# Four experts in fixed order and four ranked, with the early gates alone in the DMA queues and attention rows written into the output rows

## The reference

```
for t in range(768):                       # gated linear attention, per batch and head
    m_new = max(f[t] + m, i[t]);  fs = exp(f[t] + m - m_new);  is = exp(i[t] - m_new)
    C = fs * C + is * outer(v[t], k[t]);  n = fs * n + is * k[t]
    y[t] = sigmoid(o[t]) * (C @ q[t]) / max(|n @ q[t]|, 1)
x = y as rows                              # (3072, 320)
logits = x @ w_gate                        # 8 experts; each row goes to its argmax
out[rows of e] = softmax weight * (relu(x[rows of e] @ w1[e]) @ w2[e])     # 320 -> 1024 -> 320
h = out @ w_in;  result = max(0.01 * h, h) @ w_out                         # 320 -> 2048 -> 320
```

## Time and profile before

| | us |
|---|---|
| median of 3 runs (lowest, highest) | 835.92 (832.53, 836.61) |
| the profiled execution | 834.39 |
| its span | 832.7 |
| busy: PE / DVE / ACT / POOL | 746.0 / 531.0 / 388.3 / 146.5 |
| TensorE clock granted, mean | 0.976 of full |

### The profile page before, as it was taken

One profiled execution on the slowest core, in us unless ns is written; L12 is line 12 of the kernel. 1 busy time (PEld: TensorE's weight loads), 2 busy tenths in 40 slices (PEclk: granted clock), 3 DMA queues, 4 the chain that ended last, 5 costly groups with the idle time before them and its releaser, 6 DMA issues.

```text
span 832.7 us, 17702 instructions
## 1 busy us (share of the span) xinstructions
PE 746.0 (90%) x6435; PEld 552.7 (66%) x6436; DVE 531.0 (64%) x1382; ACT 388.3 (47%) x713; POOL 146.5 (18%) x202
## 2 busy tenths in 40 slices
PE   0798999898178899999999989999999999999994
PEld 0577888787157788887888855555555555555552
DVE  7468999898776656766476666555455465554441
ACT  2457464664625557545654323343343433433432
POOL 4334443344131111111010000020010100100101
PEclk9999999999589999999999999999999999999998
DMA  9559999992052995397540000000000000000000
GB/s 235 150 151 307 296 298 288 275 282 83 9 150 95 327 348 198 125 357 271 190 152 2 2 2 2 1 32 1 1 33 1 24 8 0 31 0 1 32 2 31
DMA packets 49401, 99.75 MB, mean 120 GB/s; under 512 B 7822, under 2 KB 38222, under 8 KB 46766
## 3 DMA queue, kind: packets, MB, share of 16 engines
q1 hardware_dynamic: 39906, 67.65, 26.9%
q10 hardware_dynamic: 6780, 22.10, 7.8%
q0 software_dynamic: 2640, 9.01, 3.2%
HBM read 74.85 MB, written 23.89 MB: 119 GB/s over the span
## 4 chain that ended last, share of the span: by engine, by line
PE 81%; DMA 6%; DVE 5%; issue 3%; SPq 2%; ACT 1%; POOL 1%; ACTq 0%; DVEq 0%
PE bank L1524 33%; PE bank L1658 19%; PE bank L1558 12%; PE bank L1391 4%; PE bank L1420 3%; DMA vv<-v_in 2%; DMA d_parts<-xreg 1%; PE bank L1412 1%; PE bank L1514 1%; PE bank L1404 1%; PE bank L1443 1%; PE bank L1381 1%; PE bank L1383 1%; DMA d_x<-og 1%; PE bank L1635 1%
## 5 line engine op out<-in xcount | busy, mean ns | idle before, releaser
L1524 PE MATMUL bank<-stage,slot 128*128 128x512 f16 x768 | 181.1, 379 | 0.0
L1658 PE MATMUL bank<-slot,dec 128*128 128x320 f16 x768 | 159.1, 299 | 0.0
L1524 PE MATMUL bank<-qbd,slot 128*128 128x128 f16 x1984 | 120.1, 223 | 11.1 <-issue 11.1
L1524 PEld LDWEIGHTS bank<-qbd,slot 128*128 128x128 f16 x1984 | 116.2, 100 | 14.2 <-issue 13.9
L1524 PEld LDWEIGHTS bank<-stage,slot 128*128 128x128 f16 x768 | 75.1, 98 | 74.3 <-DVE stage L1323 0.2
L1327 DVE TENSOR_TENSOR qk<-stage,dec 128x512 f16<-128x512 f32 x96 | 66.4, 692 | 84.8 <-ACT dec L853 84.8
L1658 PE MATMUL bank<-slot,qk 128*128 128x320 f16 x384 | 114.8, 299 | 0.0
L1323 DVE TENSOR_TENSOR stage<-bank,stage 128x512 f32<-128x512 f32 x96 | 66.2, 690 | 67.4 <-ACT stage L847 66.9
L853 ACT CAST dec<-stage 128x512 f16<-128x512 f32 x96 | 59.4, 619 | 100.7 <-PE bank L1658 72.8
L1658 PEld LDWEIGHTS bank<-slot,dec 128*128 128x128 f16 x768 | 75.1, 98 | 44.3 <-DVE qk L1327 0.2
L1558 PE MATMUL bank<-slot,emov 128*128 128x320 f16 x496 | 102.0, 299 | 2.3 <-issue 1.5
(11 more groups left out here) (260 smaller groups left out, 1126.4 us busy)
## 6 DMA issues: line engine op xcount, KB each, us to landing
slot<-d_w SPq DMA_DIRECT2D x12, 1280.0 KB, 7.0
d_w<-slot ACTq DMA_DIRECT2D x4, 2560.0 KB, 8.9
stage<-wB SPq DMA_DIRECT2D x6, 1280.0 KB, 7.2
stage<-wA SPq DMA_DIRECT2D x6, 1024.0 KB
d_w<-slot SPq DMA_DIRECT2D x4, 1280.0 KB, 8.9
stage<-wB ACTq DMA_DIRECT2D x4, 1280.0 KB, 14.3
qk<-qkT SPq DMA_DIRECT2D x12, 360.0 KB
slot<-qkT SPq DMA_DIRECT2D x12, 360.0 KB
```

The lines of the kernel that those rows point to most:

```text
L1524: ins = t_.matmul(pf, a[:, col:col + P], x(k), start=(q == 0), stop=(q == len(ops) - 1))
L1658: ins = t_.matmul(bank[4 + q][:, 0:DM], x[f % 2][:, q * P:(q + 1) * P], slotB[2 + f // NF][:, c0:c0 + DM], start=(f == 0 and z == 0), stop ...
```

## The change

- **Start.** SP issues the keys, queries and values of steps 0 and 1, then their output gates, and then waits until step 1's inputs, the exponent parts among them, have landed. Only then come the inputs of steps 2 and 3, with unit 2's first half between them, then `w_gate` and unit 2's second half. DVE's chain fills 128 columns of ones instead of 768 before it starts, and clears `esta` after the parts rather than before. POOL's clearing of the third buffer (`late_set(2)`) waits for that.
- **Rows.** From step 4 on (`EARLY = 4`) POOL writes the finished row into its own columns of `xreg`; PE reads it and SP stores it from there. The output gates of step 8 and later need only that the row is made. ACT clears `xreg` once all rows are stored.
- **Four fixed, four ranked.** `NS = 4`: experts 0 to 3 are fixed, 4 to 7 ranked. Attention converts units 2, 1 and 0 and stores unit 2 alone; unit 3 is squared in attention and converted after it; unit 4 (the first ranked one) is loaded by SP as soon as the ranking is known, and squared on ACT before the first rows are cast. DVE makes the ranking table earlier, ahead of the index work. All tables are rewritten.
- The queries' buffer `qbd` is laid out by head in the group instead of by group.

```diff
-            link(v.memset(gr0, 1.0))
+            link(v.memset(gr0[:, 0:P], 1.0))
             link(v.memset(gm0[:, 0:1], NEG))
-            for i in range(2):
-                link(v.memset(esta[i][:, :].bitcast(F32), 0.0))
-                link(v.memset(esta[i][0:3, :].bitcast(F32), TWO_ONES))
...
             parts(gp0[:, 3:6, :], gb, 1.0, 0, P)
             assert n[0] == GATE_PARTS, n[0]
+            for i in range(2):
+                link(v.memset(esta[i][:, :].bitcast(F32), 0.0))
+                link(v.memset(esta[i][0:3, :].bitcast(F32), TWO_ONES))
+            assert n[0] == GATE_SETS, n[0]
+            link(v.memset(gr0[:, P:S], 1.0))
...
+            pool.wait_ge(gate_chain, GATE_SETS)
             late_set(2)
...
             for b in range(2):
                 load_k(0, b)
-                load_o(0, b)
                 sp.wait_ge(set_done, SETS[b])
                 load_q(0, b)
                 load_v(0, b)
-            load_A(2)
-            load_B(2)
+            for b in range(2):
+                load_o(0, b)
+            sp.wait_ge(in_landed[1], landed(0, 1))
+            for b in range(2, B):
+                load_k(0, b)
+                sp.wait_ge(set_done, SETS[b])
+                load_q(0, b)
+                load_v(0, b)
+                load_e(0, b)
+                if b == 2:
+                    load_A(2)
+                load_o(0, b)
...
-            sp.wait_ge(parts_stored, 16)
-            for b in range(2, B):
...
+            load_B(2)
...
+            def load_o_late(st):
+                if st >= 2 * EARLY:
+                    sp.wait_ge(x_done, st - EARLY + 1)
+                else:
+                    sp.wait_ge(x_stored[st % NBUF], 16)
+                load_o(st // B, st % B)
...
             sp.wait_ge(rt_ord, 1)
-            sp.wait_ge(xt_landed[NX - 1], 16)
-            sp.wait_ge(lo_done, lows_until(1))
-            load_A(5)
-            load_B(5)
+            sp.wait_ge(lo_done, lows_until(0))
+            load_A(NS)
+            load_B(NS)
...
-                g.tensor_tensor(o3, num[i][:, :, 0:D], o3, ALU.mult).then_inc(x_done, 1)
+                if st == EARLY:
+                    pool.wait_ge(rest_stored, 16)
+                    pool.wait_ge(wl_copied, 1)
+                    pool.wait_ge(gate_tr, 2)
+                g.tensor_tensor(xo(st, f).rearrange("p (h d) -> p h d", h=H), num[i][:, :, 0:D], o3,
+                                ALU.mult).then_inc(x_done, 1)
...
+            act.wait_ge(pv_done, NG * NST)
+            act.wait_ge(x_done, NST)
+            for k in range(NSL):
+                high(3, k)
+            for i in range(NBUF):
+                act.wait_ge(x_stored[i], 16 * NC)
             a.copy(xreg[:, :], zero[:, :].broadcast_to([P, NST * DM])).then_inc(m_y, 1)
-            act.wait_ge(pv_done, NG * NST)
-            act.wait_ge(x_stored[2], 16 * NC)
             for k in range(NSL):
-                high(4, k)
+                square(4, k)
...
+            rl(v.tensor_tensor(tmp8, isk, iota_j[:, 0:NE].unsqueeze(1).broadcast_to(ee), ALU.mult))
+            rl(v.tensor_reduce(ordf, tmp8, AX.X, ALU.add))
+            v.tensor_scalar(tab_ord[:, NS:NE], ordf[:, NS:NE], -2.0, None, ALU.add).then_inc(rt_ord, 1)
             rl(v.tensor_tensor(shift, isk, past.unsqueeze(1).broadcast_to(ee), ALU.mult))
...
-SPLITS = (2, 3, 0, 1, 4, 5, 6, 7, 8, 9)
+SPLITS = (2, 1, 0, 3, 4, 5, 6, 7, 8, 9)
-SLOT = (0, 1, 0, 1, 2, 3, 2, 3, 2, 3)
+SLOT = (0, 1, 0, 3, 2, 3, 2, 3, 2, 3)
+LOWS = {(5, 2): (2, 0), (6, 0): (2, 1), (6, 2): (2, 2), (7, 2): (2, 3), (8, 2): (2, 4),
+        (12, 1): (1, 0), (13, 1): (1, 1), (14, 1): (1, 2), (15, 1): (1, 3), (16, 1): (1, 4),
+        (18, 1): (0, 0), (19, 1): (0, 1), (20, 1): (0, 2), (21, 1): (0, 3), (22, 1): (0, 4)}
-SUMS_AT = {3: 2, 7: 3, 12: 0, 17: 1, 22: 4}
+SUMS_AT = {4: 2, 11: 1, 17: 0, 23: 3}
-LOAD_A = {2: 3, 8: 0, 13: 1, 18: 4}
+LOAD_A = {5: 1, 11: 0, 17: 3}
-STORE_A = {6: 2, 11: 3}
+STORE_A = {8: 2}
-PAIR_SCALE = {3: 5, 9: 6, 13: 7, 23: 8}
+PAIR_SQ = {4: ((5, 0), (5, 1), (5, 2)), 5: ((5, 3), (5, 4)), 6: ((6, 0), (6, 1), (6, 2)), 9: ((6, 3), (6, 4)),
+           12: ((7, 0),), 13: ((7, 1), (7, 2)), 14: ((7, 3), (7, 4)), 17: ((8, 0),), 18: ((8, 1), (8, 2)),
+           19: ((8, 3), (8, 4)), 20: ((9, 0), (9, 1), (9, 2)), 21: ((9, 3), (9, 4))}
+PAIR_SCALE = {2: 4, 7: 5, 11: 6, 15: 7, 23: 8}
+PAIR_HI = {2: ((4, 0), (4, 1), (4, 2)), 3: ((4, 3), (4, 4)), 7: ((5, 0), (5, 1), (5, 2)), 8: ((5, 3), (5, 4)),
...
+PAIR_LO = {0: ((3, 0), (3, 1)), 1: ((3, 2), (3, 3), (3, 4)), 2: ((4, 0), (4, 1)), 3: ((4, 2), (4, 3), (4, 4)),
...
-PAIR_STORE = {2: 4, 4: 5, 13: 6, 17: 7}
-PAIR_LOAD = {3: 6, 6: 7, 14: 8, 18: 9}
+PAIR_STORE = {2: 3, 3: 4, 10: 5, 15: 6, 19: 7}
+PAIR_LOAD = {2: 5, 4: 6, 9: 7, 15: 8, 18: 9}
```

More of the change, by code:

```diff
@@ L91, in build @@
         xreg = sb("xreg", [P, NST * DM], F32)
-        qbd = [sb(f"qbd{i}", [P, NG, GH * P], F32) for i in range(2)]
+        qbd = [sb(f"qbd{i}", [P, GH, NG, P], F32) for i in range(2)]
         qk = [sb(f"qk{i}", [P, 2, NG, P], F32) for i in range(2)]
@@ L125, in build, with xo @@
         wtmp = sb("wtmp", [P, 2], F32)
+        def xo(st, j):
+            return og[j][:, :] if st < EARLY else xreg[:, st * DM:(st + 1) * DM]
         gat = xreg[0:BH, :]
@@ L253, in build @@
         xsc = [kt[i][:, :, :].rearrange("p g t -> p (g t)") for i in range(2)]
-        xh = [qbd[i][:, 0, :].bitcast(F16)[:, 0:3 * P] for i in range(2)]
-        xl = [qbd[i][:, 1, :].bitcast(F16)[:, 0:3 * P] for i in range(2)]
+        xh = [qbd[i][:, 0, :, :].rearrange("p g t -> p (g t)").bitcast(F16)[:, 0:3 * P] for i in range(2)]
+        xl = [qbd[i][:, 1, :, :].rearrange("p g t -> p (g t)").bitcast(F16)[:, 0:3 * P] for i in range(2)]
         hh = [emov[i][:, :].bitcast(F16) for i in range(2)]
@@ L402, in store_x @@
                 r0 = st % B * S + st // B * P
-                sp.dma_start(d_x[r0:r0 + P, :], og[j][:, :]).then_inc(x_stored[j], 16)
-            def load_o_late(c, b):
-                sp.wait_ge(x_stored[b], 16 * c)
-                load_o(c, b)
+                sp.dma_start(d_x[r0:r0 + P, :], xo(st, j)).then_inc(x_stored[j], 16)
+            def load_o_late(st):
[4 more added lines that the diff above has]
+                load_o(st // B, st % B)
             def reload(c, b, st):
                 inputs = not (is_c(c, NC - 1) and b >= 2)
-                gates = not (is_st(st, 2) or is_st(st, NST - 1))
+                gates = [s for s in range(EARLY, NST) if st == (s - 1 if s < 2 * EARLY else s - 2)]
                 c2, b2 = (c, b + 2) if b < 2 else (c + 1, b - 2)
@@ L425, in reload @@
                     load_e(c2, b2)
-                if gates:
-                    sp.wait_ge(tr_done, st - 2)
                 if inputs:
                     load_v(c2, b2)
-                if gates:
-                    load_o_late(*((c, b + 1) if b < B - 1 else (c + 1, 0)))
+                for s in gates:
+                    if s < 2 * EARLY:
+                        sp.wait_ge(tr_done, s - EARLY + 1)
+                    load_o_late(s)
                 if st == 2:
                     decays()
-                if st in LOAD_A and LOAD_A[st] != 3:
+                if st in LOAD_A and SPLITS.index(LOAD_A[st]) >= 2:
                     sp.wait_ge(lo_done, lows_until(SPLITS[SPLITS.index(LOAD_A[st]) - 2]))
@@ L716, in job @@
                     x, k = HIGHS[st, at]
-                    if k == 0 and x < 2:
-                        act.wait_ge(stored[x + 2], 32)
+                    if (x, k) == (0, 0):
+                        act.wait_ge(stored[2], 32)
                     high(x, k)
@@ L798, in jobs @@
                 for x, k in PAIR_HI.get(p, ()):
-                    if k == 0 and x >= NS + 1:
+                    if k == 0 and x > NS:
                         act.wait_ge(stored[x - 2], stores(x - 2))
@@ L1386, in scores @@
             def scores(u, g, f, i):
-                w = heads(g) * P
+                nh = heads(g)
                 if not (isinstance(u, int) and u < 2):
                     pe.wait_ge(p_done, u - 1)
-                t_.matmul(psS[i][:, 0:w], kt[f][0:GH * D, g, :], qbd[f][0:GH * D, g, 0:w],
+                t_.matmul(psS[i][:, 0:nh * P], kt[f][0:GH * D, g, :], qbd[f][0:GH * D, 0:nh, g, :],
                           start=True, stop=True).then_inc(s_done, 1)
@@ L1609, in _ @@
             pair(1, 1)
+            sums(NS)
             pair(2, 0)
             at = 3
-            for p in sorted(PAIR_SCALE):
+            for p in sorted(PAIR_SCALE)[1:]:
                 if p > at:
@@ L1697 @@
 CONSTS = 11
[L1698 removed]
+LATE = 1 + 4 + 6
 SETS = (3, 6, 11, 16)
 TWO_ONES = 1.0019378662109375
[L1701 removed]
+GATE_FIRST = 2 + 5
 GATE_PARTS = GATE_FIRST + 8
[L1703 removed]
+GATE_SETS = GATE_PARTS + 4
+GATE_SCAN = GATE_SETS + 1 + NC - 1 + 1 + 2 * (NC - 1) + 1
 GATE_ALL = GATE_SCAN + 8
@@ L1706 @@
 NBUF = 4
+EARLY = 4
 NSL = 5
```

52 lines of the change are left out of this document (18 added, 34 removed), and 20 rows, old and new, of tables (HIGHS, LOWS, PAIR_HI, PAIR_LO).

## The result

The changed kernel takes 842.4 us (median of 5 runs, 841.3 to 844.0) where the kernel before, run beside it, takes 835.1 (832.5 to 836.6): a ratio of 1.0094, with a 95% interval of 1.0071 to 1.0117. It is slower, where 824 was forecast. Its profiled execution took 843.7 with a span of 842.0, against 834.4 and 832.7.

What follows compares the result with a forecast made beforehand. It took the start as a DVE-store-load-PE chain, attention and experts as bound by PE, routing by a DVE chain. From 834.4, -10.3 + 0.5 - 5.5 + 2.3 + 2.5 = -10.5 gave 824 us, range 818 to 829.

Steps and rivals of the forecast that it cites:

- Start: Before attention: shorter DVE chain, store and loads let PE begin at 15.3 instead of 25.56; 10.3 us gained (7.5 to 12.5).
- What is late next: After PE's earlier start: DVE's clears and ones delay the gate chain and DVE's first product; cost 0.5 us (0 to 2).
- SP's queue: Before step 4's reload: `w_gate` and unit 2's second half queue where SP waits anyway; 0, up to 2 us.
- Waits for values: Attention: fewer transfers remove most of PE's 5.2 us of waits for a step's values; 4 us gained.
- Low parts' place: Attention: ten later low parts stand after group 1 instead of group 2; 0 to 1.4 us each, taken as 0.
- Scale chains, rows in xreg: Attention: four scale chains instead of five, 0 net (-1.4 to +1.5); POOL writing rows to another place, 0.
- Routing: Routing stage: earlier ranking operations, unit 4's late squares and its load's tail delay the row casts; cost 2.3 us (0.7 to 5).
- Expert stage: Pairs 0 to 6: added parts, and ACT stalling on stores and loads in its queue; cost 2.5 us (0 to 10).
- DVE's overfull pairs: Expert stage, pairs 0 to 3: three low parts overfill a pair by 1 us, twice, absorbed by lead; 0 to 2.
- one loop more than before: Expert stage: six loops of pairs instead of five may add one instruction fetch, 1.8 us or nothing; left out.
- ACT waits for weights in order: Rival, routing and experts: late units 4, 5 and 6 stall ACT, PE's clock falls; 21 instead of 4.8, 840; chance 0.06.
- The one rival with a loss there: Rival, attention: unit 2's 2.8 MB moving inside attention (10 us) eat the early gain; 833; chance 0.06.

Runs made afterwards that it cites:

- e5: Changed kernel without POOL's wait that holds its clearing of the third buffer; PE starts at 14.52 us, median not different from the changed kernel's beyond the intervals.
- e6: Changed kernel with SP's old order of issues at the start; PE starts 9.9 us later, attention 6.8 us shorter, whole 4.9 us longer by the medians.
- e12: Changed kernel with later low parts after group 2, units 5 and 6 squared later, unit 3 stored earlier, gates' stores earlier, decays stored first; attention 178.8 us.
- e1: Changed kernel with its ten later low parts after group 2 instead of group 1; 7.4 us shorter by the medians, 8.2 by the ratios.
- e13: e12 with unit 4's squares in pairs 0 and 1 and unit 6's store at the end of pair 14 instead of 15; 834.5 us.
- e14: e12 with the squares of units 5 and 6 back where the change put them; 826.1 us, 1.1% below the kernel before.
- e9: Changed kernel with unit 3's store at the end of pair 1 instead of pair 2; 5.1 us shorter by the medians, 6 by the ratios.
- e8: Changed kernel with PE's pairs written out instead of in loops of two; 19 us slower than the changed kernel.

## Why the prediction was wrong

Against the profiled execution before, the forecast was 10.5 us less and the measured one 9.3 us more. Of these 19.8 us attention has 13.2 (7.7 lost where 5.5 gained were forecast) and the experts' stage 8.7 (11.2 lost for 2.5); start and routing came out 2.1 us better.

- *Start, -10.3.* Right: -11.1, with PE at 14.43 for 15.3 and the store landed at 12.35 for 12.3. Its inner split was wrong: the cast's 2 us counted in the sum, and e5 shows that they are worth nothing behind the drain. 9.9 of the 11.1 us are SP's order (e6).
- *"What is late next", 0.5.* Its first part, DVE's first product, was there as described, at 18.94 for the 19 of the prediction, and mis-sized in this execution: the first row transposes come 18.2 us after PE's start where the kernel before has 16.3. The runs with the same start have 16.2 to 19.9.
- *SP's queue, 0.* Failed. The prediction looked at `w_gate`, and not at the decays' round trip through memory, whose deadline (step 4) came 11 us earlier with PE while its store stayed behind a full queue and its loads went out at 42.80. Measured: some 4 us at step 4 in the profiled execution (12.5 against 8.1 to 8.5 in e12 and e6). Runs with the same code have 8.25 to 12.4 there.
- *Waits for values, -4.* Right and a little more in the profiled execution: all 5.2 went, and a smaller one of 0.9. In the experiments with the same early code 0 to 2.3 us of them are left.
- *Low parts' place, 0, "between 0 and 1.4 each".* Failed, and the largest error: 8.2 us in ten steps, 7.4 to 8.2 of the whole (e1). Without it attention behind step 4 would be 5 us shorter than before, as forecast. The doubt was named, with 7.3 us a step as its sign, and then settled by volume ("the DVE time of a step is the same"). What mattered was which instruction stands behind the moved one on DVE and who waits for it: the copy of the logits, 1.3 to 1.5 us later, and PE's transposes behind it. The row that could have told was the wait of 1.23 us before the transposes of step 21, the one step before with a low part after group 1.
- *Scale chains, rows in xreg.* Steps with a scale, the first of each kernel aside, take 8.15 to 8.17, as 8.13 to 8.28 before: nothing to see.
- *Routing, +2.3.* Right within 0.8: +1.5. Without the squares there it is 0.7 less (e13).
- *Expert stage, +2.5 (0 to 10).* Mis-sized: +11.2. Its mechanism was named, the store and load in ACT's queue in pairs 2 to 6. The prediction counted when the data would land and took ACT's lead as cover. It did not count that the issues themselves hold ACT, 4.3 us, that this puts unit 6's load 4 to 6 us later (e14, e9), or the low clock behind each stall. One pair between store and load returns 8.0 of the 11.2 (e9). DVE's overfull pairs did not show. A part of it is no transfer at all as far as the profile tells: 4.9 us in pair 12, behind an unnamed wait of 2.39 us. It lies in the first round of the loop from pair 11. The prediction had one loop more than before at 1.8 us or nothing and left it out; that the further loop is the cause is not shown.

The measured time lies where the prediction put 0.04. The rival "ACT waits for weights in order", given 0.06 and 840, came nearest in time, partly by luck: its stalls in pairs 4 and 6 to 8 are real, but it had 21 us for the experts and routing together, which measured 12.7, and two thirds of the miss lay in attention. The one rival with a loss there put it on transfers, and PE's waits for values went; neither the low parts' place nor the decays stood in any. With the three misplaced pieces put right (e14) the sum comes out near the forecast, 826.1 and 823.3 in the profiled execution, and term by term: start -11.3, attention -4.1, routing +1.8, experts +2.4.

What stays open: the experts' stage of e14 is still 2.4 us longer than before. Pair 12 alone takes 3.5 us more than before, with an unnamed wait of 2.77 us; every run with the changed tables has one of 1.9 to 3.2 us in that pair, and nothing here tells its cause. Open too is why the first row transposes come 16.2 to 19.9 us after the same start.

## What to carry to other kernels

Where an engine is nearly full, price a move by the order and not by the volume: write down what stands behind the moved instruction and who waits for it, above all a short copy that frees a bank. When a stage is made to start earlier, list everything that had a deadline in it, the round trips through memory too, and see whether their sources started earlier as well. And don't put a large store and a large load one behind the other in the queue of an engine that has other work: issuing them holds the engine. That costs only where others wait for it soon, as in pair 4 here; in pairs 15 to 17 freeing ACT gained nothing (e13).

## What the runs showed of the hardware

- Issuing a DMA can hold its engine far longer than the usual 0.3 to 0.6 us for one: 5.50 us for three and 4.08 for one on SP behind unit 2, 2.66 for two issues and 1.66 for one on ACT behind a store of 2.6 MB, and 1.20 and 0.55 once 7 us lay between (e9). With unit 8's load it was 3.52 and 1.64 right behind a store, and 1.47 and 0.60 once 9 us lay between (e13).
- After 5.25 us without work PE ran at 0.50 of its clock for some 6 us; with two gaps of 1.08 and 1.50 us close together it did too (e13), and behind 2.39 us in pair 12 the granted clock was 0.58. The pairs with such stalls grew by 1.5 to 2.3 times the idle time. Single gaps of 1.83 and 2.08 us in pairs 15 and 17 of the changed kernel left the clock at 1.00 and cost 2.2 and 2.3 us.
- A 32x128 cast from f32 to bf16 on DVE took 2.31 us beside POOL's clearing and 0.21 to 0.30 without it (e5).
- PE's pairs written out cost more than the same pairs in loops of two: 35.4 us of unnamed waits instead of 12.5, and 18.6 us of the stage (e8).
